# Operand parts with buffers of their own, reordered products, and weight preparation moved later in a Strassen MLP kernel

## What is computed

```python
x = attention(q, k, v, mem_k, mem_v)                      # 3072 x 512
h = np.maximum(np.maximum(x @ w1, x @ w2), x @ w3)        # 768 wide
y = h @ w_out
h2 = y @ w_in                                             # 2048 wide
g = np.where(h2 >= 1, h2, np.where(h2 <= -1, 0, (h2 + 1) ** 2 / 4))
out = g @ w_out2
```

## Time and profile before

| | us |
|---|---|
| runs before | 1017.90, 1017.11, 1016.00 |
| median | 1017.11 |
| the profiled execution | 1021.69 |
| its span, first to last instruction | 1019.9 |
| PE busy in the span | 958.8 |
| POOL busy in the span | 419.4 |
| mean granted clock of TensorE | 0.973 |

### The profile page before, as it was taken

One profiled execution on the slowest core, in us unless ns is written; L12 is line 12 of the kernel. 1 busy time (PEld: TensorE's weight loads), 2 busy tenths in 40 slices (PEclk: granted clock), 3 DMA queues, 4 the chain that ended last, 5 costly groups with the idle time before them and its releaser, 6 DMA issues. The chain is left out here.

```text
span 1019.9 us, 18893 instructions
## 1 busy us (share of the span) xinstructions
PE 958.8 (94%) x7806; PEld 888.4 (87%) x7806; DVE 479.6 (47%) x728; ACT 440.5 (43%) x722; POOL 419.4 (41%) x535
## 2 busy tenths in 40 slices
PE   5999975988998989899999999999999999999998
PEld 4999975888997979798988989889988899889897
DVE  4754571845736646365135443254433444332331
ACT  3433331422433324343245545655546455464454
POOL 2768994766628473300033232332332323323321
PEclk9999996997999889999999999999999999999999
DMA  9778877999849684667444555546446344473431
GB/s 358 265 279 271 319 251 255 370 349 353 295 161 387 253 331 156 239 212 263 152 154 169 180 174 173 183 158 215 147 165 220 141 166 130 152 244 115 165 114 62
DMA packets 39110, 222.99 MB, mean 219 GB/s; under 512 B 4465, under 2 KB 8561, under 8 KB 31473
## 3 DMA queue, kind: packets, MB, share of 16 engines
q0 software_dynamic: 20720, 165.16, 45.3%
q1 hardware_dynamic: 18304, 56.63, 15.7%
HBM read 178.00 MB, written 43.78 MB: 217 GB/s over the span
## 5 line engine op out<-in xcount | busy, mean ns | idle before, releaser
L561 PE MATMUL mlp_ps<-yc,wi 128*128 128x384 f32 x826 | 286.4, 347 | 45.6 <-DMA wi<-wi_scratch 38.8
L827 ACT ACTIVATE up_m<-mlp_ps 128x384 f32<-128x384 f32 x302 | 147.6, 490 | 345.1 <-PE mlp_ps L563 338.9
L562 PE MATMUL mlp_ps<-yc,wi 128*128 128x384 f32 x826 | 282.7, 342 | 0.0
L563 PE MATMUL mlp_ps<-yc,wi 128*128 128x384 f32 x826 | 281.5, 341 | 0.0
L561 PEld LDWEIGHTS mlp_ps<-yc,wi 128*128 128x128 f32 x826 | 159.2, 193 | 60.6 <-DMA wi<-wi_scratch 42.2
L562 PEld LDWEIGHTS mlp_ps<-yc,wi 128*128 128x128 f32 x826 | 159.5, 193 | 8.8
L563 PEld LDWEIGHTS mlp_ps<-yc,wi 128*128 128x128 f32 x826 | 159.2, 193 | 0.0
L468 POOL DMA_DIRECT2D wi<-wi_scratch x59 | 31.4, 533 | 276.6 <-PE mlp_ps L563 276.6
L491 POOL CAST wo<-wo_raw 128x1024 fp32r<-128x1024 f32 x32 | 33.3, 1040 | 208.0 <-PE trans_ps L563 201.9
L1438 DVE SCALAR_TENSOR_TENSOR ramp<-ramp,up_m 128x768 f32<-128x768 f32 x64 | 61.5, 961 | 112.4 <-ACT ramp L1095 112.4
L1432 DVE TENSOR_TENSOR up_m<-up_m 128x384 f32<-128x384 f32 x32 | 19.8, 620 | 163.9 <-ACT up_m L827 163.9
(11 more groups left out here) (165 smaller groups left out, 1822.4 us busy)
## 6 DMA issues: line engine op xcount, KB each, us to landing
wi<-wi_scratch POOLq DMA_DIRECT2D x59, 1792.0 KB, 7.7
wi_scratch<-stage_a POOLq DMA_DIRECT2D x29, 896.0 KB, 6.2
qk_raw<-qk_l SPq DMA_DIRECT2D x24, 768.0 KB, 7.6
wo_raw<-w_out POOLq DMA_DIRECT2D x32, 512.0 KB, 3.8
v_raw<-v_l SPq DMA_DIRECT2D x24, 512.0 KB, 6.3
y_scratch<-up_m SPq DMA_DIRECT2D x32, 192.0 KB, 2.1
y_raw<-y_scratch SPq DMA_DIRECT2D x8, 768.0 KB, 4.9
out<-out_stage SPq DMA_DIRECT2D x24, 256.0 KB, 3.4
```

The source lines that it names most:

```text
L561: pe.matmul(out_ap, a_hi, b_hi, start=first, stop=False, skip_group_check=beside)
L562: pe.matmul(out_ap, a_lo, b_hi, start=False, stop=False, skip_group_check=beside)
L563: return pe.matmul(out_ap, a_hi, b_lo, start=False, stop=last, skip_group_check=beside)
L827: return act.activation(o, i, ACT.Copy)
```

## The change

**Two parts per pair.** The seven weight operands of an item are stored, kept and loaded in two parts, operands 0 to 3 (1024 KB, `wa`) and 4 to 6 (768 KB, `wb`), each with its own pair of buffers, its own HBM scratch and its own semaphores. The first layer takes its products in the order `PRODUCTS_S`, in which products 0 to 3 use part a and products 4 to 6 part b. Part a of period g + 2 is loaded when product 3 of period g is done, part b when product 6 is done. In the second MLP the order of the products is as before, `product(g, 0)` waits for both parts, and both are loaded where `load_wi` was.

**The banks and sums follow the new order.** There are four snapshots and four block sums per pair (the fourth block's copy by ACT, `last_block`, and the place `m5` are gone for the first layer). DVE makes block sums 2 and 3 behind product 6, then the maxima of blocks 2 and 3. At the end of a tile DVE runs `block_max` for blocks 2 and 3 and then `h2_low` for all four blocks; `l2_product(v, 0)` now starts with t = 0 and waits at its fifth f for three of these (before: `block_max` of block 3 and then `h2_low` for three blocks).

**The halves.** A half is `split_begin` (sums, high copies) and `split_end` (low differences, two stores, next raw load), with the load of part a between them in the first layer. The plan of the halves is written out: 12 before the first Strassen tile (before: 14); 12 to 17 in periods 0 to 5; 20 and 21 in periods 11 and 14; 24 to 27 in periods 19, 21, 23, 25; 18, 19 and 22, 23 at the ends of tiles 0 and 1, where the second layer runs; and 28 to 33 two at a time in the first three periods of the second MLP, with buffers of their own, after the wait for `l2_done`. Before, all were done by period 19 of the first layer.

```diff
-EARLY, AHEAD = 5, 14
-Y_ORDER = (0, 3, 1, 2)
-H_ORDER = ((0, 0), (1, 1), (0, 1), (1, 0))
+EARLY, AHEAD, LAST_PAIR, LATE = 4, 12, 24, 28
+HALF_IN = {0: 12, 1: 13, 2: 14, 3: 15, 4: 16, 5: 17, 11: 20, 14: 21, 19: 24, 21: 25, 23: 26, 25: 27}
+HALVES_IN_L2 = {0: (18, 19), 1: (22, 23)}
+WA_COLS, WB_COLS = 4 * 2 * P, 3 * 2 * P
+H_ORDER = ((0, 0), (0, 1), (1, 0), (1, 1))
...
+PRODUCTS_S = ((W_A11, Y_B11), (W_A22, Y_T4), (W_S1, Y_T1), (W_A12, Y_B21), (W_S2, Y_T2), (W_S4, Y_B22), (W_S3, Y_T3))
...
-            return mlp[(g + (0, 1, 0, 2, 0, 2, 0)[i]) % 3][:, 0:TT]
+            return mlp[(g + (0, 1, 2, 1, 0, 2, 0)[i]) % 3][:, 0:TT]
...
-            return x // 2, 1 - x % 2
+            return x // 2, x % 2
...
             def load_raw(n):
...
-                if n >= 2:
+                if n > LATE:
+                    pool.wait_ge(w_split, 2 * n)
+                elif n >= 2:
                     pool.wait_ge(w_split, 2 * (n - 1))
...
+            def split_end(n):
...
                 pool.wait_ge(w_hi_done, 2 * n + 1)
+                pool.tensor_tensor(lo_a, raw, hi_a, ALU.subtract).then_inc(w_split, 1)
                 pool.wait_ge(w_hi_done, 2 * n + 2)
+                pool.tensor_tensor(lo_b, sums, hi_b, ALU.subtract).then_inc(w_split, 1)
+                if n >= 2:
+                    pool.wait_ge(w_stored[j], 32 * item)
+                pool.wait_ge(w_split, 2 * n + 1)
+                pool.dma_start(wa_scratch[item][:, j * WA_COLS:(j + 1) * WA_COLS], both[:, 0:WA_COLS]).then_inc(w_stored[j], 16)
                 pool.wait_ge(w_split, 2 * (n + 1))
+                pool.dma_start(wb_scratch[item][:, j * WB_COLS:(j + 1) * WB_COLS], both[:, WA_COLS:W_COLS]).then_inc(w_stored[j], 16)
+                if n + 2 < LATE:
                     load_raw(n + 2)
...
             for n in range(AHEAD):
-                split_half(n)
+                split_begin(n)
+                split_end(n)
             pool.wait_ge(mlp_done, TG + L1G)
-            load_wi(0)
-            load_wi(1)
+            for n in range(2):
+                load_wa(n)
+                load_wb(n)
             for g in range(PERIODS_S):
-                if AHEAD + g < 2 * ITEMS:
-                    split_half(AHEAD + g)
+                n = HALF_IN.get(g)
+                if n is not None:
+                    split_begin(n)
+                pool.wait_ge(l1_done, 7 * g + 4)
+                load_wa(g + 2)
+                if n is not None:
+                    split_end(n)
                 pool.wait_ge(l1_done, 7 * (g + 1))
-                load_wi(g + 2)
+                load_wb(g + 2)
+                if (g + 1) % PAIRS_S == 0:
+                    for n in HALVES_IN_L2.get(g // PAIRS_S, ()):
+                        split_begin(n)
+                        split_end(n)
...
             pool.wait_ge(l2_done, 2 * KD * TILES_S)
             load_wo(0)
+            load_raw(LATE)
             for g in range(PERIODS):
+                late = [n for n in (LATE + 2 * g, LATE + 2 * g + 1) if n < 2 * ITEMS]
+                for n in late[0:1]:
+                    split_begin(n)
+                    split_end(n)
+                    load_raw(n + 1)
                 split_wo(g)
                 if g + 1 < PERIODS:
                     pool.wait_ge(wo_split, 2 * (g + 1))
                     load_wo(g + 1)
+                for n in late[1:2]:
+                    split_begin(n)
+                    split_end(n)
+                    if n + 1 < 2 * ITEMS:
+                        load_raw(n + 1)
                 if g + 2 < PERIODS:
                     pool.wait_ge(prod_done, 7 * (g + 1))
-                    load_wi(PERIODS_S + g + 2)
+                    load_wa(PERIODS_S + g + 2)
+                    load_wb(PERIODS_S + g + 2)
...
+                    pe.wait_ge(wa_in[g % 2], 16 * (g // 2 + 1))
+                if i == 4:
+                    pe.wait_ge(wb_in[g % 2], 16 * (g // 2 + 1))
+                if q == 0 and i < 2:
+                    pe.wait_ge(x_split, 8 * v + (6, 8)[i])
...
+                elif q and i < 3:
+                    pe.wait_ge(summed, 4 * (g - 1) + (1, 2, 4)[i])
+                elif i >= 3:
+
+                    pe.wait_ge(snapped, 4 * g + (0, 0, 0, 2, 1, 3, 4)[i])
...
                 elif g:
-                    act.wait_ge(merged, merges(g - 1) + (1, 0, 3, 0, 2)[i])
+                    act.wait_ge(merged, merges(g - 1) + b + 1)
...
+                    if i == 6:
+                        block_sum(g, 2)
+                        block_sum(g, 3)
                     if attention and r == 0:
                         softmax_shift(n, n % GT, n // GT)
                     if attention and r == 3:
                         softmax_scale(n, n % 2, prob[:, n % 2])
-                    if i == 1:
+                    if i == 0 and q and (q - 1) % 3:
+                        block_max(g - 1, 2)
+                        block_max(g - 1, 3)
...
-                block_max(PAIRS_S * (v + 1) - 1, 3)
-                for b in range(1, 4):
+                for b in range(2, 4):
+                    block_max(PAIRS_S * (v + 1) - 1, b)
+                for b in range(4):
                     h2_low(KFP * (v + 1) - 1, b)
```

More of the change, by code:

```diff
@@ L129, in build_attention_and_two_mlps @@
         yc1 = sbuf(second, "yc1", [2, 2, Y_COLS], F32R)
-        wi0 = sbuf(second, "wi0", [2, 2, W_HALF], F32R)
-        wi1 = sbuf(second, "wi1", [2, 2, W_HALF], F32R)
+        wa = [sbuf(second, f"wa{i}", [2, 2, 4 * P], F32R) for i in range(2)]
+        wb = [sbuf(second, f"wb{i}", [2, 2, 3 * P], F32R) for i in range(2)]
         second.close()
@@ L444, in split_half @@
                 pool.tensor_tensor(s4, a12, s2, ALU.subtract).then_inc(w_sums_done, 1)
[L445 to L451 removed]
+                last = staged_last(n)
```

207 lines of the change are left out of this document (89 added, 118 removed).

## The result

| | before | after |
|---|---|---|
| median of 8 runs each, side by side | 1016.57 us (1014.6 to 1018.79) | 1022.43 us (1019.09 to 1024.2) |
| ratio after to before, 95% interval | | 1.0061 (1.0045 to 1.0077) |
| profiled execution, its span, mean granted clock | 1021.69, 1019.9, 0.973 | 1023.23, 1021.4, 0.980 |

A forecast was written before the change was run, and what follows sets the result against it. TensorE sets the time, losing 18 us in the gap and 43 in the tiles to late loads. Gain 45 minus second-MLP loss 32 gives 13: 1008.7 profiled, 1004 for the median, range 986 to 1017.

The forecast's parts named there:

- The gap: Before the first Strassen tile: first product starts at 148.5 instead of 164.9, 16.4 us won.
- Waits for weights in tiles 0 and 1: First-layer tiles: earlier requests give 11 to 13 us for 1 MB; no weight wait above 1 us in tiles 1 and 2.
- Tile ends: Ends of tiles 0 and 1: seven VectorE operations, 3.9 us, against cover of 2.1; 2 us lost, twice.
- Tile 2: Third Strassen tile: of 9.5 us lost before, nearly all should go; its end is covered by two second-MLP products.
- The forecast's 10 us: Losses left in the tiles: DMA backlog 2, VectorE late behind product 6 4, VectorE beside POOL 2.5, half-clock stretches 1.5.
- The term "2.5 us": In the tiles: VectorE sharing memory access with POOL stretches single operations, 2.5 us in all.
- The second MLP: Two late halves ahead of each load on POOL delay periods 2 to 4; 32 us lost, bounds 22 to 42.
- The rule of the Trainium skill: Second MLP: 2.0 us fixed per DMA, if serial, adds 6 us over three loads, leaving a gain of 7; not adopted.
- The slower one: Rival: late halves beside VectorE cost 2.7 us more each, raw loads 5 in all; 53 against 45, time 1025; chance 0.12.
- The first tile bound by DMAs: Rival: first tile stays DMA-bound at 370 GB/s or first loads land late; 10 us less gain, 1014; chance 0.15.
- The hidden rival: Rival, second MLP: late halves mostly run in POOL's idle time, loss about 10, time 982; chance 0.07.
- The prediction's own signs of being wrong: Wrong if second-MLP period 4 starts within 10 us of its old place against T, or last second layer ends after 480.

The follow-up runs named there:

- Experiment 8: Kernel before with only experiment 2's plan of halves (12 ahead, none in the second MLP), operands in one part: 1001.29 us, ratio 0.9862 to before.
- experiment 6: experiment 2 with POOL holding the halves at the ends of tiles 0 and 1 until VectorE has made its low parts: 988.26 us, one run.
- Experiment 5: experiment 2 with no halves in tile 2, halves in all nine periods of tile 0, three in each second layer: 987.81 us, ratio 0.9728 to before.
- experiment 2: Changed kernel with all halves, including 28 to 33, made in the first MLP and none in the second: 989.08 us, ratio 0.9715 to before.
- experiment 11: experiment 2 with a shorter VectorE chain at tile ends, and split_end of a half released one product later: 978.72 us, ratio 0.9625 to before.
- experiment 4: Changed kernel with the six late halves one per period instead of two in the second MLP: 994.49 us, ratio 0.9767 to before.

## Why the prediction was wrong, step by step

The sign was wrong: 1004 was forecast, within 986 to 1017, and 1022.4 came. Of the 18.4 us, 10.3 are a gain in the first MLP that was sized too high, 4.2 a loss in the second sized too low, and the rest, 3.8 or so, is how profile and median stand to each other: I took 4.6 off for a profiled execution above its median, and the one of after is 0.8 above.

- **The gap** held: first product at 148.65, 148.5 forecast. Experiment 8 shows that it belongs to the plan of halves alone.
- **Waits for weights in tiles 0 and 1** held: the kernel after has none there. What was to stay of other kinds, in all three tiles, was 10 us; tiles 0 and 1 take 88.7 and 81.7 against an undisturbed 80.1 each, 10.2 in all (the 80.1 is an estimate from the fastest periods with attention in the traces).
- **Tile ends: mis-sized.** "2 us lost, twice" was 4.2, twice. The wait is 2.78, where the same operations without POOL beside them give 1.39 (experiment 6), and the half-speed stretch behind it adds about 1.6. I had counted the seven operations at their undisturbed 0.55 us and left the clock out, though the first tile had shown that it falls behind long waits.
- **Tile 2: left out.** The forecast's 10 us are used up by tiles 0 and 1; tile 2 lost another 73.9 - 65.5 = 8.4. About 3.2 are three waits for VectorE, 1.0, 0.5 and 1.7, and 2.8 a wait at its end, for part b of the second MLP's first period, whose load POOL issued at 444.44 behind half 27's subtractions; some 2 stand in no wait that the trace names:

```profile
453.14 0.41 PE L622 MATMUL mlp_ps<-yc,wa 128*128 128x384 f32 x1 [2.82 <-DMA wb<-wb_scratch]
```

  The forecast gave part b eleven products from its request to its use. Here it had seven, since the second MLP's first product waits for both parts: period 25 ended at 442.97, period 26 at 450.31, and the load, issued 1.5 us late, landed 8.45 us after its issue.

  The term "2.5 us" for VectorE beside POOL failed because I priced a collision by the few stretched rows of the kernel before, where a half starts when a period does, and did not see that the change ties two engines' work to the same event, the end of product 3. The longest maximum went from 1.55 to 2.96 us. Experiment 5 shows that the halves are to blame (for 5.4 of the 6.1 us of experiment 2), experiment 11 that their moment is, for 4 us of the whole but only 1.3 in tile 2: of the three waits the 1.0 is gone there, the 0.5 and the 1.7 stay. Together with the tile ends' 4.4 that is 12.8 too much kept; 2.6 come off, because by the same count the tiles of before lost 45.6 and not 43.
- **A typical profile: not seen.** The traced execution of before spent 6.4 us more up to T than its second trace. I took one sample of what a chain of late loads costs as what is there to be won. Against the second trace the first MLP's gain is 508.6 - 480.3 = 28.3 us.
- **The second MLP** held in its mechanism: period 2 at T + 35.5 (35 forecast), the wait before the first down 6.2 (5), waits of 7.7, 7.3 and 7.4 (11, 7, 7). The size came out 36.2 instead of 32: a cycle is 24.9 and 24.5 us instead of 23.8, twice 0.9, and the half-clock stretches after every wait cost more than the one that I counted; period 4 alone took 18.3 us instead of 15.6. About 1 us of it is a slip in the sum: loads at T + 73 that land after 9.7 us put period 4 near T + 82.5 and not at 81.5; it began at T + 85.0. Here POOL's order decides, and experiments 2 and 4 confirm it: without late halves the loss is gone, with one a period it is 10 us.
- **The rule of the Trainium skill.** Paid in series, a second load's fixed 2.0 us (the Trainium skill, "DMA: Bandwidth & Descriptors", "Anatomy of one DMA — SWDGE (gpsimd) path") would by an estimate have put period 2 near T + 37 and later ones 2 us further each; it began at T + 35.5. The two loads' landings overlap:

```profile
wa<-wa_scratch POOLq DMA_DIRECT2D x59, 1024.0 KB, 5.2
wb<-wb_scratch POOLq DMA_DIRECT2D x59, 768.0 KB, 6.6
```

  Of the three late pairs the second landed 8.8, 8.8 and 8.3 us after the first was issued, where the forecast allowed 9.7. From 600 to 900 us, where both are issued together and nothing is late, it is 7.0 by the medians, against 7.6 for the one load of before.

- **The rivals.** The slower one had the sign and not the reason. It wanted each late half 2.7 us longer beside VectorE. The first one is 7.26 us from its start to its store (486.21 to 493.47), the others 5.57, 5.16, 6.61, 5.17 and 6.98: 3.1 more in six than at 5.6, where it wanted 16. The first tile bound by DMAs shows a share of 0.98 at 362 GB/s, near the forecast's 370, and lost 8.6 us over the undisturbed 80.1; the second tile, at 0.79, lost 1.6. But no wait of PE in either tile is for a load, so this rival isn't shown. The hidden rival fell with experiment 2; of late halves at one per period all but the first would be hidden, as experiment 4 shows.
- **The prediction's own signs of being wrong.** One came, by little: the last second layer ended after 480, at 480.3. The other did not: period 4 started 33.6 us later against T, and not within 10.

What stays open: most of the 8.6 us of tile 0, whose waits for softmax, block sums and copies are 2.3, 2.0 and 1.0 us, and to which one stretch of 3.4 us at the lower clock adds; where the halves' cost in tile 2 comes from beyond the waits named; and whether the late halves would be free behind the loads.

## What to carry to other kernels

On an engine that issues loads in order, work put ahead of a load delays it one for one as soon as the engine's idle time is used up, so a plan of such pieces must be counted period by period against the engine's idle time, and that one piece fits (experiment 4) doesn't mean that two do (the kernel after). Where a change gates two engines by the same event, look whether both then touch SBUF at once; one product's delay on the side that has time was worth 0.4 to 0.7%. Before a gain is counted from waits in one trace, look at how much of it a second trace shows.

## What the runs showed of the hardware that was not expected

- VectorE's maximum of two SBUF operands, 128x384, stands still while POOL subtracts with two SBUF operands: 2.96 us beside 1.31 + 1.01, instead of 0.56. Its sums with one operand in PSUM, on the same event and as large, are never stretched:

```profile
L1343 DVE TENSOR_TENSOR up_m<-up_m,mlp_ps x108: 537/547/555, 153.9 to 450.8; 128x384 f32<-128x384 f32 x108
```

  The low parts (`h2_low`), also of two SBUF operands, reach 2.90 us. The Trainium skill, "GPSIMD Engine Reference", "Key points", says that GpSimd shares its SBUF interfaces with VectorE and that VectorE's instructions with two SBUF inputs contend. Here the trace agrees and gives the size, up to the whole length of POOL's two operations, five times the maximum's own time. In all seven long cases the maximum started first, 0.2 to 0.3 us ahead of POOL's first subtraction, and ended 0.4 us behind its second.
- A wait of 2.78 us of TensorE was followed by a stretch at 1.2 GHz, 3.4 us at a mean of 0.50, in which PE does what takes 1.7 at full clock; the same place with a wait of 1.39 us was not. In the second MLP the waits of 6.2 to 7.7 us were each followed by one. The length of the wait alone doesn't decide it: in the same kernel one of 1.79 us in tile 0, at 200.75, was followed by such a stretch from 202.2 on, and one of 2.82 us, at the end of tile 2, was not:

```profile
453.10:457.10 4.00, 3.96 (x23) 1.00 0.50 186
```

- Splitting a load of 1792 KB in 1024 and 768 KB brought the first part in 5.2 us and the second in 6.6 (medians of all issues, each from its own), against 7.7 for the whole.
